# First channel-mixing layer by seven block products (Strassen) in place of eight, weights split per step

## The chip, the core and the metric

One NeuronCore of a Trainium2 chip runs the whole program. Its engines work side by side and meet only through semaphores: TensorE (PE: matmuls, whose stationary operand is loaded by a separate weight load, PEld), VectorE (DVE), ScalarE (ACT), GpSimd (POOL), and SyncE (SP), which here issues every DMA. The metric is the device time of one execution in microseconds, lower is better. Before the change the median of three runs is 671.56 us (671.55 to 672.13).

## The reference

Batch 4, 576 tokens, model width 512. Windowed causal attention (8 heads of 64, window 64) feeds a gated MLP with spatial mixing, and that feeds a mixer. The last lines are where the change lies:

```python
def _moe2_ref(x, w_tok1, w_tok2, w_ch1, w_ch2):      # x: 4 x 576 x 512
    xt = x.transpose(0, 2, 1)
    h = np.maximum(xt @ w_tok1, 0.0) @ w_tok2        # token layers
    u = x + h.transpose(0, 2, 1)
    h2 = np.maximum(u @ w_ch1, 0.0) @ w_ch2          # 512 -> 1536 -> 512
    return u + h2
```

## The kernel before, in words

Work runs in segments: a prologue, one segment for each batch but the last, and an epilogue. In each, the attention of one batch is woven into the MLP and token layers of the batch before. The order on each engine is written out by hand in tables of short names (`PROLOGUE_PE`, `LOOP_DVE`, `ALL_SP`, ...), which the engines' streams walk through. In the tables for PE, `g` is spatial mixing, `y` the projection, `t` transposes, `a` and `b` the two token layers. After the epilogue comes the channel stage, the two layers with w_ch1 and w_ch2 over all 4 x 576 = 2304 tokens. It has no other work beside it.

Every large matmul is made in three passes over operands that are split in a high part (rounded to fp32r) and a low part (what is left): high by high, high by low, low by high. The helper `product` (line 1158) issues these three matmuls. The high part is made by ACT (a copy with the rounding), the low part by DVE or POOL (a subtraction).

The channel stage before the change takes 384 tokens at a time, 6 chunks. Its weights are loaded and split once, during the last segment and the epilogue: 14 pieces, `wb0` to `wb13` in the tables (ACT `channel_high` L825, POOL `channel_low` L690, SP L587), and held in the arena. In a chunk, for each of the 12 blocks j of 128 hidden features, `hidden` makes 4 x 3 matmuls of 384 columns in bank 6 or 7; ACT takes relu and rounds (L833), DVE makes the low part (L1080, one input from PSUM, one from SBUF). Then 3 x 3 matmuls of 512 columns add the block's share to three output tiles. PE runs two j ahead of the second layer (`H0`, `H1` in the epilogue's table are the first two). At the end of a chunk DVE adds the residual rows to each tile (L1146) and SP stores it (L619). The residual `u` is held in DRAM twice: `u2_dram` (columns, u_scratch in the profile) and `rows_dram` (rows, u_rows), written by SP at the end of each batch (`st`, L565, and `sr`, L580, four DMAs for each of four m). SP waits for all of these to have landed before it loads the first residual rows (L607).

Of the kernel before, what the change touches and what calls it, by code (L numbers as in the profile page):

```python
# [20 lines left out]
P = 128  # L21
# [4 lines left out]
def bass_attention_gmlp_mixer_kernel(nc, q, k, v, w_in, w_spatial, b_spatial, w_out, w_tok1, w_tok2, w_ch1, w_ch2, out):  # L26
# [21 lines left out]
    def tile_of(blk):  # L48
# [36 lines left out]
    PROLOGUE_DVE = (
        "ke0 m0 vo1 m1 ke1 r0 ke2 r1 m2 m3 hv0 hv1 r2 c0 c1 r3 m4 c2 hv2 hu0 c3 hu1 ke3 r4 m5 lv0 xl0 hv3 c4 vo2 "
        "r5 lv2 wl0 m6 c5 m7 xl1 hu2 hu3 r6 wl1 vs0 xl2 vo3 vn0 r7 c6 m8 wl2 wl3 vl0 r8 vs1 c7 vo4 c8 vs2 wl4 xl3 "
        "vn1 kt0 vn2 xl4 vl1 kt1 vl2 vs3 vs4 wl5 vn3 vn4 vl3 vl4").split()
    FIRST_DVE = (
# [4 lines left out]
        "vs4 vn3 ut2 vl3 ut3 vn4 kt0 vl4 kt1").split()  # L94
    LOOP_DVE = (
# [88 lines left out]
    with ctx:  # L184
# [528 lines left out]
        def _(act):  # L713
# [121 lines left out]
            for kind, b, x, _ in ACT_ORDER:  # L835
# [30 lines left out]
                elif kind == "H":  # L866
                    hidden(0, x)
# [582 lines left out]
```

## Time and profile before

| | us |
|---|---|
| median of three runs | 671.56 |
| profiled execution, its own time | 672.14 |
| its span, first to last instruction | 670.2 |
| PE busy | 657.2 |
| DVE, ACT, POOL busy | 317.8, 228.0, 150.0 |

Lines of the profile name engine, line of the kernel, operation, output<-input, shape and count. The span in 40 slices (16.75 us each) has PE at 9 (90% or more) in every slice but the first and the last, and the granted clock at 9 throughout. From about 375 us on POOL is idle, DVE and ACT are busy to one or two tenths. A matmul's busy time is longer than the distance to the next, since they are pipelined, so what a matmul costs is read from the starts of groups.

### The profile page before, as it was taken

Reading aid. Unit: us, or ns where it says so; the run is one execution under the profiler, and the core shown is the slowest. Engines: PE = TensorE matmul, PEld = TensorE weight load, DVE = VectorE, ACT = ScalarE, POOL = GpSimd, SP = SyncE. Lnnn points to the kernel's source line nnn. Section 1 sums busy time; section 2 is a strip of 40 time slices with the busy share of each in tenths; the row PEclk is TensorE's granted clock in tenths of the full one; section 3 lists DMA queues with packets and bytes.
Section 4 is the critical chain, followed back from the end, with each engine's and each line's share of the span. In section 5 each row is a group of like instructions: output and inputs, shape, how many; then the busy total and the mean of one; then the engine's idle time right before and its main releaser. Section 6 shows DMA issues by size and latency. Waiting matters only on the chain.

```text
span 670.2 us, 11369 instructions
## 1 busy us (share of the span) xinstructions
PE 657.2 (98%) x4025; PEld 609.0 (91%) x4025; DVE 317.8 (47%) x893; ACT 228.0 (34%) x642; POOL 150.0 (22%) x237
## 2 busy tenths in 40 slices
PE   6899999999999999999999999999999999999997
PEld 5799999999999999998999999999999999999996
DVE  4887887678675887747534221221221221221211
ACT  4775356334563344633356111111111111111110
POOL 3560437411234212343348200000000000000000
PEclk9999999999999999999999999999999999999999
DMA  9838164586435864436931720400300400400101
GB/s 245 208 60 156 32 180 117 116 177 129 108 103 120 175 121 107 113 87 146 291 97 67 162 86 1 142 0 1 141 0 0 141 0 0 142 0 1 48 0 48
DMA packets 169362, 64.82 MB, mean 97 GB/s; under 512 B 126304, under 2 KB 157600, under 8 KB 169312
## 3 DMA queue, kind: packets, MB, share of 16 engines
q1 hardware_dynamic: 169312, 64.17, 37.5%
q8 instruction: 29, 0.48, 0.3%
q14 instruction: 21, 0.17, 0.1%
HBM read 42.91 MB, written 21.23 MB: 96 GB/s over the span
## 4 chain that ended last, share of the span: by engine, by line
PE 96%; DVE 1%; DMA 1%; issue 1%; POOL 0%; ACT 0%; SPq 0%; POOLq 0%; DVEq 0%
PE ps L1158 71%; PE ps L1259 13%; PE ps L1228 5%; PE ps L1198 4%; PE ps L1322 1%; DMA prob_blocks<-att 1%; PE ps L1177 1%; DVE att L930 0%; PE ps L1208 0%; DMA att<-prob_blocks 0%; PE ps L1247 0%; DVE att L1146 0%; ACT xT L753 0%; ACT att L723 0%; SPq L575 0%
## 5 line engine op out<-in xcount | busy, mean ns | idle before, releaser
L1158 PE MATMUL ps<-arena 128*128 128x288 f32 (+3 forms) x2064 | 352.0, 324 | 0.0
L1158 PEld LDWEIGHTS ps<-arena 128*128 128x128 f32 (+1 forms) x2064 | 323.8, 186 | 18.4
L1158 PE MATMUL ps<-arena,att_r 128*128 128x512 f32 x648 | 161.1, 393 | 0.0
L1080 DVE SCALAR_TENSOR_TENSOR att_r<-ps,att_r 128x384 fp32r<-128x384 f32 x72 | 40.1, 557 | 226.2 <-ACT att_r L833 226.1
L1158 PEld LDWEIGHTS ps<-arena,att_r 128*128 128x128 f32 x648 | 120.6, 188 | 22.0
L833 ACT ACTIVATE att_r<-ps 128x384 fp32r<-128x384 f32 x72 | 35.4, 492 | 251.1 <-PE ps L1158 251.1
L1259 PE MATMUL ps<-arena 128*128 128x288 f32 (+1 forms) x560 | 89.3, 316 | 0.0
L1259 PEld LDWEIGHTS ps<-arena 128*128 128x128 f32 x560 | 80.2, 188 | 3.9
L661 POOL TENSOR_SCALAR att<-att,rinv 128x128 f32<-128x128 f32 x144 | 54.4, 399 | 118.6 <-DVE rinv L941 118.5
L743 ACT ACTIVATE att<-att,nmax 128x128 f32<-128x128 f32 x144 | 55.8, 390 | 7.1 <-DVE nmax L930 6.7
L1228 PE MATMUL ps<-att 128*128 128x128 f32 x288 | 37.2, 276 | 2.1 <-DVE att L950 1.1
L1198 PE MATMUL ps<-att 128*128 128x128 f32 x288 | 38.5, 282 | 0.8 <-DVE att L904 0.7
L1228 PEld LDWEIGHTS ps<-att 128*128 128x128 f32 x288 | 35.1, 191 | 3.1 <-DVE att L950 1.3
L930 DVE CUSTOM_DVE_ANT_0 att<-ps,mask 128x128 f32<-128x128 f32 x144 | 33.3, 286 | 9.6 <-PE ps L1198 7.6
L1198 PEld LDWEIGHTS ps<-att 128*128 128x128 f32 x288 | 36.1, 198 | 1.2 <-DVE att L904 1.0
L753 ACT ACTIVATE xT<-ps 64x256 f32<-64x256 f32 x72 | 27.1, 376 | 24.3 <-PE ps L1228 23.8
L690 POOL TENSOR_TENSOR arena<-att,arena 128x768 fp32r<-128x768 f32 (+1 forms) x14 | 29.3, 2115 | 26.4 <-ACT arena L825 26.4
L743 ACT ACTIVATION_READ_ACCUMULATOR att<-att,nmax 128x1 f32 x144 | 27.1, 188 | 0.0
L667 POOL TENSOR_TENSOR rstd<-veps,mhalf 128x1 f32<-128x1 f32 (+1 forms) x20 | 14.5, 726 | 49.3 <-DVE veps L1006 49.1
L913 DVE STREAM_TRANSPOSE att<-att 64x256 f32<-64x256 f32 x54 | 23.6, 436 | 3.7 <-DMA att<-in_q_dram 3.1
L959 DVE STREAM_TRANSPOSE att<-att 128x512 f32<-128x512 f32 x27 | 19.1, 707 | 12.8 <-PE ps L1228 11.8
L799 ACT ACTIVATE arena<-gate 128x288 fp32r<-128x288 f32 x32 | 13.6, 438 | 32.5 <-DVE gate L1041 32.4
(77 smaller groups left out, 433.5 us busy)
## 6 DMA issues: line engine op xcount, KB each, us to landing
prob_blocks<-att SPq DMA_DIRECT2D x27, 256.0 KB, 2.6
att<-prob_blocks SPq DMA_DIRECT2D x108, 64.0 KB, 2.0
u_scratch<-uy SPq DMA_DIRECT2D x16, 288.0 KB, 2.7
att<-u_rows SPq DMA_DIRECT2D x18, 256.0 KB, 4.8
out_dram<-att SPq DMA_DIRECT2D x18, 256.0 KB, 2.1
att<-in_v_dram SPq DMA_DIRECT2D x16, 256.0 KB, 3.7
att<-in_k_dram SPq DMA_DIRECT2D x48, 72.0 KB, 2.5
att<-in_q_dram SPq DMA_DIRECT2D x48, 72.0 KB, 2.5
```

The costliest lines, as they stand in the source:

```text
L661: ins = pool.tensor_scalar(x, x, rinv[:, g % 3, p:p + 1], 1.0, ALU.mult, ALU.mult)
L690: pool.tensor_tensor(lo, staged(c, hi), hi.bitcast(F32), ALU.subtract).then_inc(w_ready, 1)
L743: ins = act.activation(x, x, ACT.Exp, bias=nmax[:, g % 3, p:p + 1], scale=-1.0, accum_out=psums[:, g % 3, p:p + 1])
L753: ins = act.activation(xT3[c, :, blk * WINDOW:(blk + 1) * WINDOW], tp[c, bank, :].rearrange("p (w h n) -> p w h n", w=PAIRS, h=2)[:, :, h, ...
L833: act.activation(h3[:, j % RING, 0, :], ps[:, 6 + j % 2, 0:CK], ACT.Relu).then_inc(h_hi, 1)
L913: ins = dve.transpose(qd[c, g // 2 % 2, g % 2, :, h, :], qn[c, :, blk * WINDOW:(blk + 1) * WINDOW])
L930: ins = dve.tensor_tensor_reduce(out=prob[:, g % 3, P * p:P * (p + 1)], in0=ps[:, 4 + g % 2, P * p:P * (p + 1)], in1=mask[:, 0:P] if blk e ...
L1080: dve.scalar_tensor_tensor(out=h3[:, j % RING, 1, :], in0=ps[:, 6 + j % 2, 0:CK], scalar=0.0, in1=h3[:, j % RING, 0, :].bitcast(F32), op0= ...
L1158: ins = pe.matmul(dst, w[a], x[c], start=first and n == 0, stop=last and n == 2, skip_group_check=True)
L1198: ins = pe.matmul(ps[:, 4 + g % 2, P * p:P * (p + 1)], qd[:, g // 2 % 2, g % 2, p].rearrange("p h n -> p (h n)"), kT[:, p, at:at + P], sta ...
L1228: ins = pe.matmul(tp[:, bank, P * p:P * (p + 1)], window[:, P * p:P * (p + 1)], keys[:, p], start=True, stop=True)
L1259: ins = pe.matmul(dst, d, w, start=t == 0 and n == 0, stop=t == NT - 1 and n == len(pairs) - 1, skip_group_check=True)
```

## The change

The channel stage takes 768 tokens at a time (`s`, three of them), seen as two halves of 384, and the 1536 hidden features as six pairs (`i`) of 128-feature blocks, one from each half. The 512 inputs are two halves of 256. So each step n = 6s + i (18 steps) is a 2 x 2 by 2 x 2 block product, made by seven products of sums of blocks in place of eight (Strassen, in Winograd's form: 4 sums of weights, 4 sums of data, 7 sums of results of which 4 are gathered in PSUM by leaving `start` off). One product is 2 x 3 matmuls of 384 columns. PE does the first layer of step n woven with the 12 second-layer products (3 matmuls of 512 columns each) of step n-1.

- Weights: SP loads step n+1's w_ch1 blocks when the seven products of step n-1 are done, and w_ch2's block of step n when the second layer of step n-2 is done. Each step DVE makes 4 sums (128x256, `weight_sums`), ACT rounds 128x1792 (`weight_high`) and 128x1024 (`second_high`), POOL makes their low parts (`weight_low`, `second_low`). Nothing is held.
- Data: once for each s, in the steps before it, DVE makes 4 sums (128x768, `data_sum`, two each in steps i = 1 and 2), ACT rounds 7 pieces, POOL makes 7 low parts of 128x768 (`data_low`).
- Results: ACT copies three part results out of bank 6 (`copy_part`), DVE adds them to bank 7 (`add_part`), ACT takes relu and rounds (`hidden_high`), DVE makes the low part (`hidden_low`). For j = 0, 1, 3 its two inputs are now both in SBUF.
- Output: six tiles for each s, in banks 0 to 5. `add_rest` has three buffers for residual rows: the load of row tile r waits for the sum of tile r-3.
- The tables of the first four stages are written anew too, and the stage's hardware loops are unrolled.

```diff
     EPILOGUE_PE = (
-        "... a0 t2 t3 a1 t4 a2 a3 a4 H0 b00 b10 b20 b30 b01 b11 b21 b31 H1").split()
+        "... a0 t2 t3 a1 t4 a2 a3 a4 P0 P1 b00 b10 b20 b30 b01 b11 b21 b31 P2 P3 P4 P5 P6").split()
     EPILOGUE_ACT = (
+        "... xe6 ah0 ah1 pc0 pc1 pc2 he0 he1 he2 he3").split()
     EPILOGUE_DVE = (
+        "... al0 al1 cs0 te00 te10 te20 te30 te01 te11 te21 te31 ut0 ut1 ut2 cs1 ut3 cs2 dh0 dh1 dh2 dh3").split()
     EPILOGUE_POOL = (
-        "wb0 wb1 wb2 wb3 wb4 wb5 wb6 wb7 uf0 wb8 wb9 wb10 wb11 wb12 wb13").split()
+        "xo0 xo1 ao0 xo2 xo3 ao1 xo4 xo5 xo6 wo0").split()
...
+        SLOT_A, SLOT_X, SLOT_BANK = (0, 1, 4, 5, 3, 6, 2), (0, 1, 4, 5, 3, 2, 6), (0, 1, 0, 1, 0, 0, 1)
+        OPENS = (True, True, False, True, False, False, False)
+        AFTER_SLOT = (2, 2, 2, 1, 2, 2, 1)
+        UNIT_TILE = (0, 1, 2, 3, 4, 5, 3, 4, 5, 0, 1, 2)
...
         @block.sync
+            for n in range(1, NW + 1):
+                if n + 1 < NW:
+                    sp.wait_ge(first_done, 7 * n)
+                    load_weights(n + 1)
+                if n < NW:
+                    if n >= 2:
+                        sp.wait_ge(second_done, 12 * (n - 1))
+                    load_second(n)
+                if n == 1:
+                    sp.wait_ge(*unit_full(("acc_a", B - 1, KT - 1)))
+                if n in (1, NI):
+                    sp.wait_ge(xc_sum, 4 * (n // NI + 1))
+                    for x in range(4):
+                        load_data(n // NI + 1, x)
+                if n % NI == 4:
+                    for t in range(3):
+                        load_rest(n // NI * 6 + t)
+                if n % NI == 0:
+                    for t in range(6):
+                        store((n // NI - 1) * 6 + t)
+                        if t < 3:
+                            load_rest((n // NI - 1) * 6 + t + 3)
...
         @block.gpsimd
+            for n in range(1, NW):
+                s, i = divmod(n, NI)
+                second_low(n)
+                if n + 1 < NW:
+                    weight_low(n + 1)
+                if s + 1 < NS:
+                    for k in ((), (), (), (0, 1), (2, 3, 4), (5, 6))[i]:
+                        data_low(s + 1, k)
...
         @block.scalar
+                copy_part(n, 0)
+                hidden_high(n, 0)
+                second_high(n)
+                copy_part(n, 1)
+                if n + 1 < NW:
+                    weight_high(n + 1)
+                copy_part(n, 2)
+                hidden_high(n, 1)
+                hidden_high(n, 2)
+                if s + 1 < NS:
+                    for k in ((), (), (0, 1), (2, 3, 4), (5, 6), ())[i]:
+                        data_high(s + 1, k)
+                hidden_high(n, 3)
...
         @block.vector
+                    add_part(n, 0)
+                    if n + 1 < NW:
+                        weight_sums(n + 1)
+                    hidden_low(n, 0)
+                if s + 1 < NS and i in (1, 2):
+                    data_sum(s + 1, 2 * i - 2)
+                    data_sum(s + 1, 2 * i - 1)
+                if i == 0:
+                    add_rest(r)
+                if n < NW:
+                    add_part(n, 1)
...
         @block.tensor
+            def first_product(n, k):
+                bank = ps[:, 6 + SLOT_BANK[k], 0:CK]
+                if k == 0:
+                    pe.wait_ge(a_lo, n + 1)
...
+                        pe.wait_ge(h_lo, 4 * (n - 1) + 3)
+                if k == 1 and n > 0:
+                    pe.wait_ge(total_done, 3 * (n - 1) + 3)
+                if k in (2, 4, 5):
+                    pe.wait_ge(part_copied, 3 * n + (1, None, 2, 3)[k - 2])
+                if k in (3, 6):
+                    pe.wait_ge(total_done, 3 * n + (1 if k == 3 else 2))
...
+                for i in range(2):
+                    ins = product(bank, [a[n % 2][:, SLOT_A[k], i] for a in (a_hi_at, a_lo_at)],
+                                  [x_at[n // NI % 2][:, SLOT_X[k], s, i] for s in range(2)], OPENS[k] and i == 0, i == 1)
+                ins.then_inc(first_done, 1)
...
+            for n in range(1, NW):
+                u = 0
+                for k in range(7):
+                    first_product(n, k)
+                    for _ in range(AFTER_SLOT[k]):
+                        second_product(n - 1, u)
+                        u += 1
+            for u in range(12):
+                second_product(NW - 1, u)
```

Two places in the order of the instructions matter for the prediction. The first is SP at the end of the epilogue, up to the first loads of the channel stage; each row is a line of the kernel, a transfer, its shape and the semaphores it waits for. Before:

```order
L580 DMA u_rows<-gate 32x18x32 [waits u2_turned]
L580 DMA u_rows<-gate 32x18x32 x3
L565 DMA u_scratch<-uy 128x576 [waits acc_dve] x2
L607 DMA att<-u_rows 128x512 [waits rows_stored2,u2_stored2,u2_stored3,rows_stored1,rows_stored3,u2_stored1,w_ready,rows_stored0,u2_stored0]
L607 DMA att<-u_rows 128x512 x2
```

And now, with `front` as the home of raw weights and `early` as that of raw data:

```order
L579 DMA u_rows<-gate 32x18x32 x3
L564 DMA u_scratch<-uy 128x576 [waits acc_dve] x3
L591 DMA front<-in_moe_w_ch_dram 128x4x128 [waits rows_stored2,u2_stored2,u2_stored3,rows_stored1,rows_stored3,u2_stored1,first_done,rows_stored0,u2_stored0]
L592 DMA front<-in_moe_w_ch_dram 128x2x128
L593 DMA front<-in_moe_w_ch_dram 128x2x128
L597 DMA front<-in_moe_w_ch_dram 128x2x512
L586 DMA early<-u_scratch 128x2x384 [waits xc_sum,acc_full]
L586 DMA early<-u_scratch 128x2x384 x2
L586 DMA xT<-u_scratch 128x2x384
```

The transfers that stood behind the last stores were residual rows for the end of the first chunk; now they are the weights of step 2, w_ch2's block of step 1 and the data of the second 768 tokens.

The second place is DVE in the channel stage. Before, one chunk, the last but one:

```order
L1080 SCALAR_TENSOR_TENSOR att_r<-ps,att_r 128x384 x4
L1076 TENSOR_TENSOR arena<-uy,arena 128x1536
L1080 SCALAR_TENSOR_TENSOR att_r<-ps,att_r 128x384 x8
L1146 TENSOR_TENSOR att<-ps,att 128x512 x3
```

Now, step 1 (L1173 `add_part`, L1162 to L1167 `weight_sums`, L1178 `hidden_low`, L1149 and L1151 `data_sum`):

```order
L1173 TENSOR_TENSOR vr<-ps,xT 128x384
L1162 TENSOR_TENSOR front<-front 128x256
L1163 TENSOR_TENSOR front<-front 128x256
L1165 TENSOR_TENSOR front<-front 128x256
L1167 TENSOR_TENSOR front<-front 128x256
L1178 SCALAR_TENSOR_TENSOR arena<-vr,arena 128x384
L1149 TENSOR_TENSOR early<-xT,early 128x768
L1151 TENSOR_TENSOR early<-early,xT 128x768
L1173 TENSOR_TENSOR vr<-ps,xT 128x384
L1178 SCALAR_TENSOR_TENSOR arena<-vr,arena 128x384
L1178 SCALAR_TENSOR_TENSOR arena<-ps,arena 128x384
```

Two data sums, with both inputs in SBUF, stand between the first and the second `add_part`; in steps without them `hidden_low` is followed by `add_part` directly.

## Rows read from the trace of the kernel before

**Rows 1.** The page: PE's busy time, and the chain that ended last by engine
```profile
PE 657.2 (98%) x4025; PEld 609.0 (91%) x4025; DVE 317.8 (47%) x893; ACT 228.0 (34%) x642; POOL 150.0 (22%) x237
PE 96%; DVE 1%; DMA 1%; issue 1%; POOL 0%; ACT 0%; SPq 0%; POOLq 0%; DVEq 0%
```

**Rows 2.** Groups by line and shape, PE, whole span: count, busy us, mean ns
```profile
L1158 PE MATMUL ps<-arena 128*128 128x384 f32 x864 | 163.0, 337 | 0.0
L1158 PE MATMUL ps<-arena,att_r 128*128 128x512 f32 x648 | 161.1, 393 | 0.0
```

**Rows 3.** Timeline, PE, into the channel stage: start us, us, engine, line, shape, count
```profile
359.05 12.79 PE L1158 MATMUL ps<-arena 128*128 128x384 f32 x84
371.68 2.24 PE L1158 MATMUL ps<-arena,att_r 128*128 128x512 f32 x9
373.76 2.27 PE L1158 MATMUL ps<-arena 128*128 128x384 f32 x12
375.87 2.24 PE L1158 MATMUL ps<-arena,att_r 128*128 128x512 f32 x9
```

**Rows 4.** Timeline of the end: last matmuls, residual sums, stores
```profile
660.56 6.32 PE L1158 MATMUL ps<-arena,att_r 128*128 128x512 f32 x27
665.66 2.05 DVE L1146 TENSOR_TENSOR att<-ps,att 128x512 f32<-128x512 f32 x3 [3.82 <-PE ps L1158]
666.38 1.69 SPq L619 DMA_DIRECT2D out_dram<-att  x3
```

**Rows 5.** Timeline of SP issues around the first residual loads
```profile
375.41 2.21 SPq L580 DMA_DIRECT2D u_rows<-gate  x4
377.71 0.96 SPq L565 DMA_DIRECT2D u_scratch<-uy  x2
380.92 1.31 SPq L607 DMA_DIRECT2D att<-u_rows  x3
```

**Rows 6.** Transfers: KB each and median us to landing; L607's min/median/max
```profile
att<-in_moe_w_ch_dram SPq DMA_DIRECT2D x6, 512.0 KB, 3.9
DMA to landing us min/median/max: 3.0/3.3/3.5
```

**Rows 7.** Groups by line and shape, ACT, DVE and POOL: count, busy us, mean ns
```profile
L833 ACT ACTIVATE att_r<-ps 128x384 fp32r<-128x384 f32 x66 | 32.5, 492 | 233.7 <-PE ps L1158 233.7
L829 ACT ACTIVATE arena<-uy 128x1536 fp32r<-128x1536 f32 x2 | 3.0, 1482 | 0.0
L1080 DVE SCALAR_TENSOR_TENSOR att_r<-ps,att_r 128x384 fp32r<-128x384 f32 x66 | 36.8, 557 | 214.4 <-ACT att_r L833 214.4
L1076 DVE TENSOR_TENSOR arena<-uy,arena 128x1536 fp32r<-128x1536 f32 x3 | 5.3, 1758 | 5.8 <-ACT arena L829 5.8
L690 POOL TENSOR_TENSOR arena<-att,arena 128x1024 fp32r<-128x1024 f32 x6 | 14.2, 2404 | 1.8 <-ACT arena L825 1.8
L694 POOL TENSOR_TENSOR arena<-xT,arena 128x1536 fp32r<-128x1536 f32 x1 | 3.5, 3510 | 0.2 <-ACT arena L829 0.2
```

**Rows 8.** Timelines of POOL and DVE in the epilogue, side by side in time
```profile
327.84 4.04 POOL L690 TENSOR_TENSOR arena<-att,arena 128x768 fp32r<-128x768 f32 x2 [1.60 <-ACT arena L825]
...
328.68 0.46 DVE L1034 TENSOR_TENSOR gate<-ps,bias 128x288 f32<-128x288 f32 x1 [0.53 <-PE ps L1259]
329.06 1.12 DVE L1047 TENSOR_TENSOR arena<-gate,arena 128x288 fp32r<-128x288 f32 x1
330.11 2.08 DVE L1041 TENSOR_TENSOR gate<-gate,uy 128x288 f32<-128x288 f32 x1
332.59 0.46 DVE L1041 TENSOR_TENSOR gate<-gate,uy 128x288 f32<-128x288 f32 x1
```

**Rows 9.** Windows: us, PE busy (count), granted clock, DMA share, GB/s
```profile
5.00:25.00 20.00, 15.58 (x105) 1.00 1.14 285
667.00:669.00 2.00, 0.00 (x0) 1.00 0.88 337
669.00:670.00 1.00, 0.00 (x0) 0.82 0.29 113
```

More of the change, by code:

```diff
@@ new lines, in bass_attention_gmlp_mixer_kernel @@
+        x_raw = [a.rearrange("p (c s k n) -> p c s k n", c=7, s=2, k=2) for a, _ in x_all]
+        x_at = [a.rearrange("p (c s k n) -> p c s k n", c=7, s=2, k=2) for _, a in x_all]
+        x_12 = xT[:, 0:XC].rearrange("p (k n) -> p k n", k=2)
+        part = [xT[:, XC + i * CK:XC + (i + 1) * CK] for i in range(3)]
+        total = [vr[:, 0, 0:CK], vr[:, 1, 0:CK], xT[:, XC + 3 * CK:XC + 4 * CK]]
+        h_at = arena[:, START["xhl"]:START["xhl"] + 8 * CK].rearrange("p (j s n) -> p j s n", j=4, s=2)
@@ L650, in _ @@
             pool.memset(mhalf[:, :], -0.5).then_inc(const_set, 1)
-            for i in range(4):
-                pool.sem_inc(o_stored[i], 16)
             pool.wait_ge(const_set, NCONST)
@@ new lines, in add_part, with hidden_low @@
+            def add_part(n, x):
+                dve.wait_ge(part_copied, 3 * n + (1, 3, 2)[x])
+                apart(dve)
+                dve.wait_ge(first_done, 7 * n + (2, 4, 7)[x])
+                dve.tensor_tensor(total[x], ps[:, 7, 0:CK], part[(0, 2, 1)[x]], ALU.add).then_inc(total_done, 1)
+            def hidden_low(n, j):
+                dve.wait_ge(h_hi, 4 * n + j + 1)
+                src = ps[:, 6, 0:CK] if j == 2 else total[(0, 1, None, 2)[j]]
+                dve.scalar_tensor_tensor(out=h_at[:, j, 1], in0=src, scalar=0.0, in1=h_at[:, j, 0].bitcast(F32),
+                                         op0=ALU.max, op1=ALU.subtract).then_inc(h_lo, 1)
@@ L1084, in _, with add_rest @@
+            def add_rest(r):
+                dve.wait_ge(rest_in[r % 3], 16 * (r // 3 + 1))
+                if r >= 4:
+                    dve.wait_ge(o_stored[r % 4], 16 * (r // 4))
+                apart(dve)
+                dve.wait_ge(second_done, 12 * (r // 6 * NI + NI - 1) + 6 + r % 6 + 1)
+                dve.tensor_tensor(osb[r % 4], ps[:, OUT_BANK[TILE_DONE[r % 6]], :], rest[r % 3], ALU.add).then_inc(o_copied, 1)
             for kind, b, x, _ in DVE_ORDER:
@@ L1124, in _ @@
                     turn_residual(b, x)
-                elif kind == "H":
-                    hidden(0, x)
+                elif kind == "xs":
+                    data_sum(0, x)
+                elif kind == "as":
+                    weight_sums(x)
+                elif kind == "cs":
+                    add_part(0, x)
+                elif kind == "dh":
+                    hidden_low(0, x)
                 elif kind[0] == "h":
@@ new lines, in second_product @@
+            def second_product(n, u):
+                j, tile = u // 3, UNIT_TILE[u]
+                bank = OUT_BANK[tile]
+                if u % 3 == 0:
+                    pe.wait_ge(h_lo, 4 * n + j + 1)
+                    apart(pe)
+                if u == 0:
+                    pe.wait_ge(w2_lo, n + 1)
+                    apart(pe)
+                if n == 0 and u < 6:
+                    if bank in (4, 5):
+                        pe.wait_ge(masked, BL * B)
+                    else:
+                        pe.wait_ge(*unit_free(LAST_IN[bank]))
+                elif n % NI == 0 and u < 6:
+                    pe.wait_ge(o_copied, 6 * (n // NI - 1) + TILE_DONE.index(tile) + 1)
+                c = slice(tile % 3 * P, tile % 3 * P + P)
+                ins = product(ps[:, bank, :], [h_at[:, j, s, c] for s in range(2)], [w[n % 2][:, j % 2] for w in (w2_hi_at, w2_lo_at)],
+                              n % NI == 0 and u < 6, n % NI == NI - 1 and u >= 6)
+                ins.then_inc(second_done, 1)
```

460 lines of the change are left out of this document (226 added, 234 removed), and 26 rows, old and new, of tables (ALL_SP, FIRST_DVE, LOOP_DVE).

## Prediction

> **What bounds the kernel now.** I read the page first: PE is busy 98% of the span, and the chain that ended last lies on PE for 96% of it [rows 1]. So time falls only by matmuls that go, and rises by every microsecond for which PE is made to wait. Then the groups by shape: the channel stage is 864 matmuls of 384 columns and 648 of 512 [rows 2]. Their mean durations (337 and 393 ns) are not their price, as they overlap; the timeline gives it. Nine of 512 columns start at 371.68 and the next group at 373.76, so 0.231 us each; twelve of 384 take to 375.87, so 0.1755 us each [rows 3]. 864 x 0.1755 + 648 x 0.231 = 301.3 us, and with the 48 short matmuls woven in (about 6.3 us) this is the whole of 359.05 to 666.80, where the last 27 end (660.56 + 27 x 0.231) [rows 3, 4]. There is no hole in the stage. Outside it PE's only large idle time is between 5 and 25 us, 20.0 - 15.6 = 4.4 us [rows 9].
>
> **What is removed.** Seven products for eight: 18 steps x 7 x 6 = 756 matmuls of 384 columns in place of 864. 108 x 0.1755 = **-18.9 us**. The second layer keeps its 648. The long splitting of held weights in the epilogue goes too, but lay beside PE and gives nothing.
>
> **The step.** A product (6 matmuls) takes 1.05 us, a second-layer product (3) 0.69 us, a step 7 x 1.05 + 12 x 0.69 = 15.7 us. By the order 2, 2, 2, 1, 2, 2, 1 of second products behind the slots, and counting from the step's start: slot k0 ends at 1.05, k1 at 3.5, k2 at 5.9, k4 may start at 9.1 and ends at 10.1, k5 may start at 11.5, k6 at 13.9 and ends at 15.0. The other engines have this to do in it, with ACT's copy or relu 0.49, DVE's low part or sum 0.56 from PSUM, a 256-wide sum in SBUF 0.44, a 768-wide one 0.97 (0.46 for 288 and 1.76 for 1536, between them on a line) [rows 7, 8], ACT 1.0 for 1024 and 1.7 for 1792, POOL 2.40 for 1024, 3.51 for 1536, so 2.17 ns an element and 4.07 for 1792, 1.85 for 768 [rows 7]:
> - SP issues the weights at about -0.5; a quarter MB lands 3.0 to 3.5 us after its issue, half an MB 3.9 [rows 6]. w_ch1 is there at about 4.0, w_ch2 at 4.9.
> - DVE: first sum with bank 7 at 3.7 to 4.3, four weight sums to about 6.1, then the low part of j = 0.
> - ACT: relu to 4.9, rounds w_ch2 to 6.0, copies k2's result to 6.5 (PE wants it at 9.1), rounds w_ch1's seven pieces to 8.3, copies k4's result 10.3 to 10.8 (PE wants it at 11.5).
> - POOL: 2.40 from about 6.1, then 4.07, to 13.1. PE wants these weights at 15.7.
> So a plain step hides all of it, the least room being 0.7 us at k5 (a PE-ACT-PE path) and 2.6 us at the weights. I count the plain steps at **0**, and the two with six residual sums as well (their loads at 3.0 us arrive within 1 us of their use). If the cover goes, all is paid 17 times; that is a rival below.
>
> **DVE behind POOL.** The trace shows what happens when DVE has an operation with two SBUF inputs while POOL runs a subtraction: at 330.11 one of 0.46 us took 2.08 and ended at 332.19, just after POOL's pair at 331.88; one at 329.06 took 1.12, let in between the pair. One with an input from PSUM at 328.68 took its 0.46 beside POOL [rows 8]. Now `data_sum`, `weight_sums` and three of four `hidden_low` have both inputs in SBUF. In steps i = 1 and 2 (n = 1, 2, 7, 8) DVE has, before its second `add_part`, a low part (0.56) and two data sums (0.97 each), and POOL meanwhile 2.40 and 4.07. Taking turns from 6.1 they end at 6.1 + 2.5 + 6.5 = 15.1, less 0.14 for each of three waits (of 1.77 us that POOL still ran, the 330.11 operation lost 1.63) = 14.6. `add_part` ends at 15.2, and slot k6, which waits for it, starts at 15.2 or 15.3 in place of 13.9: 1.3 us. Steps 2, 7 and 8: **+3.9 us** (bounds 0, if DVE gets all its turns first or is never held, and 5.7 at 1.9 each).
> The Trainium skill, "SBUF - State Buffer", section "Who interferes with whom", says that a DVE instruction with two SBUF inputs and a GpSimd one that reads SBUF exclude each other, and whoever started first holds the shared ports for the whole instruction. The trace agrees in kind; taken strictly (no 0.14 back) this term would be 5.1.
>
> **The turn into the stage.** Slots P2 to P6 have no second product between them. They start where the b matmuls end, 359.05 + 12 x 0.1755 + 6.3 = 367.5. P5 waits for ACT's copy of P4's result (0.2 + 0.49 + 0.1 against nothing: 0.8 us). P6 ends at 373.6; slot k0 of step 1 waits for three low parts, which on DVE stand behind the sum of P6: 0.2 + 0.56 + 3 x 0.56 + 0.1 = 2.5. Step 1 starts at 376.1.
> Its supply is late, for SP is a queue. It still has sixteen row stores, the last issued at 375.41 + 2.2 = 377.6, then now three column stores in place of two (0.57 apart), the last at 378.9; the one at 378.3 landed before the load at 380.92 [rows 5]. So step 2's weights are issued at 381.5, not at 373.8; w_ch1 lands at about 385.8, w_ch2's block for step 1, issued at 383.2, at 386.9 [rows 6]. ACT stands at w_ch2 and behind it is the copy for k4: 386.9 + 1.0 + 0.5 = 388.5, while PE was ready at 376.1 + 9.1 = 385.2. On POOL and DVE the same turns begin at 388.0: 2.40 + 4.07 + 0.97 + 0.97 - 0.14, then `add_part` 0.56, so k6 starts at 396.9 and the step ends at 398.6. Without waits steps P2 to 1 would end at 367.5 + 5.3 + 15.7 = 388.5. **+10.1 us** (bounds: 3.3, if only P5 and k0 wait; 12, if w_ch2 lands 2 us later). In the trace before this place was dense, because weights were held and only residual rows, needed 12 blocks later, stood behind the stores.
>
> **The end.** Residual rows of the last three tiles wait for buffers. Counted from the start of the last 12 second products, the first three sums end at 5.8, 6.5 and 7.2. SP issues store and load in turns 0.6 apart: loads at 6.4, 7.6, 8.8, each landing 3.0 later [rows 6], the last sum 11.85 to 12.5, and its store and the end 2.5 behind (667.7 to 670.2, the third store of rows 4). PE ends at 8.3, so the tail is 6.7 us where it was 670.2 - 666.8 = 3.4 [rows 4]. **+3.3 us** (bounds 0 and 5).
>
> **The stages before it.** The rewritten tables move the same matmuls. There is 4.4 us to win in 5 to 25 us [rows 9] and nothing elsewhere; the second half of w_in is now loaded first and the first half behind two more loads, which could cost as much. I take **0** (bounds -4.4 and +3). In the epilogue the sums lie on DVE between gate operations; POOL starts on data only after the last data sum (about 347), works 27 us, and each slot's piece is ready before its slot. 0.
>
> **Sum.** -18.9 + 3.9 + 10.1 + 3.3 = -1.6 us. From the profiled execution's 672.1 that is 670.5; the median of the runs is 0.6 lower (671.56), so I forecast 670.0.
>
> **Rivals.**
> 1. *DVE is not held in the channel stage* (it gets its turns first, or its data sums finish before POOL starts). Then the 3.9 goes and step 1's k6 starts about 3.5 earlier: 670.0 - 7.4 = 662.6. For: DVE is idle two thirds of a step. Against: rows 8. 15%.
> 2. *PE's clock falls in the turn.* PE idles 2.5, 3.3 and 3.5 us within 20 us. At the end of the trace, after its last matmul at 666.8, the granted clock is full to 669 and falls between 669 and 670 [rows 9]. If it falls before step 1's k6, the matmuls behind run at half of 2.4 GHz until it rises; with a cost of about 3 us: 673.0, slower. It decides if the idle stretch before k6 is no shorter than that one. Against: two stretches of it are broken by matmuls. 20%. The Trainium skill ("TensorE: Matmul & The Clock Gate", "Why this matters for your kernels") warns against long idle gaps between bursts of matmuls; by it this rival would be likelier.
> 3. *The weights' path is longer than a step*: loads that land 1 to 2 us later put DVE's last weight sum behind POOL, the rounding behind that, and the low part of j = 2, which slot k0 waits for, 0.4 us past the step's end. 14 steps x 0.4 = 5.6: 675.6, slower. For: 512-byte rows in these loads, and a page median of 3.9 us for larger ones. Against: 2.6 us of room at the weights. 15%.
> 4. *The new tables* gain or lose 3 us in the first four stages: 667 or 673. 15%.
>
> **Numbers.** The forecast's own case has 35%, with a range of its own of 667 to 673. A measurement here tells 0.2% (1.3 us) from no change. Faster by more: 20 of the 35, 15 of rival 1, 2 of 2, 7 of 4, so 0.44. Within: 12, 8, 1 and 3, so 0.24. Slower: 3, 10, 14 and 5, so 0.32. The range reaches to rivals 1 and 3 with their bounds: 661.5 to 678.
>
> **What would show it.** Right: 1404 matmuls in the stage; plain steps of 15.7 us; PE idle before slot k6 in steps 1, 2, 7 and 8, released by an `add_part` that ends just after a 4.07 us POOL row; PE idle before k4 of step 1, released by ACT; first w_ch1 load of the stage near 381.5; a tail near 6.7 us. Wrong: PE waiting in plain steps, a granted clock below full between 376 and 400, or a stage that starts at another time than 359.

## The result: slower by 0.8%

The changed kernel took 676.93 us (median of 5 runs, 674.58 to 678.26), the kernel before 671.56 (5 runs, 671.08 to 672.13): ratio 1.0076, 95% interval 1.0055 to 1.0097. The forecast was 670.0. The profiled execution took 676.68 us at a span of 674.7 (before: 672.1 at 670.2), so the profiles differ by 4.5 us and the medians by 5.4. Differences are read from the spans of the profiled executions.

The page of the kernel after; against [rows 1], PE is busy 13 us less in a span 4.5 us longer, and its clock row, full throughout before, has two slices of 8 in the channel stage and one at the end:

```profile
span 674.7 us, 11567 instructions
PE 643.8 (95%) x3917; PEld 590.7 (88%) x3917; DVE 403.8 (60%) x1026; ACT 297.8 (44%) x733; POOL 272.9 (40%) x279
PEclk9999999999999999999999889999999999999998
PE 84%; DMA 4%; DVE 4%; issue 3%; SPq 2%; ACT 1%; POOL 0%; DVEq 0%; POOLq 0%
front<-in_moe_w_ch_dram SPq DMA_DIRECT2D x18, 512.0 KB, 4.8
early<-u_rows SPq DMA_DIRECT2D x18, 256.0 KB, 4.5
```

The chain of waits, 96% on PE before, is now 84%, with DMA, DVE and SP's queue in it. The last two rows are issues with their median landing: 4.8 us where I had counted 3.9, 4.5 where I had counted 3.0 [rows 6].

The matmuls went as they should: 756 of 384 columns and 648 of 512, against [rows 2]. The groups by shape for PE in the channel stage (count, busy us, mean ns, idle ahead and its releasers), then the waits of the same stretch (us in total, times, longest):

```profile
L1277 PE MATMUL ps<-arena 128*128 128x512 f32 x648 | 172.1, 398 | 0.2 <-DVE front L1187 0.2
L1277 PE MATMUL ps<-att_r,arena 128*128 128x384 f32 x504 | 102.3, 339 | 9.7 <-ACT xT L887 5.8 <-DVE arena L1178 2.3 <-DVE vr L1173 1.6
L1277 PE MATMUL ps<-arena 128*128 128x384 f32 x252 | 51.0, 337 | 3.9 <-ACT xT L887 2.6 <-DVE arena L1178 0.9 <-DVE vr L1173 0.5
```

```profile
PE ps L1277 <- ACT xT L887: 8.4, 4, 2.7
PE ps L1277 <- DVE arena L1178: 3.2, 3, 2.1
PE ps L1277 <- DVE vr L1173: 2.1, 2, 1.6
```

A stage that had no wait has 14 us of them in nine places. From the starts of the trace's matmul groups I worked out the length of every step. Twelve of the steps 2 to 17 take 15.69 us, which is the dense length (no wait, full clock), and step 14 is within 0.05 of it. The rest, in us (the last row counts from 0.231 us behind the start of the last matmul):

| place | after | dense | excess |
|---|---|---|---|
| P2 to the end of step 1 | 32.1 | 21.0 | 11.1 |
| step 7 | 20.28 | 15.69 | 4.6 |
| step 8 | 16.49 | 15.69 | 0.8 |
| step 13 | 18.91 | 15.69 | 3.2 |
| last matmul to span end | 8.55 | 3.5 (before) | 5.0 |

With -18.95 for the products and -1.3 for a stage that began at 357.77 and not 359.05 this makes +4.5, the difference of the spans.

**Step 7.** PE is busy for all of step 6 and for 16.61 of the 20.28 us of step 7, both at the full clock, and the DMA engines' busy share in step 7 is 0.38. PE's and ACT's timelines in step 7:

```profile
489.34 6.85 PE L1277 MATMUL ps<-arena 128*128 128x384 f32 x33 [2.57 <-ACT xT L887]
...
487.76 1.06 ACT L883 ACTIVATE arena<-front 128x1024 fp32r<-128x1024 f32 x1 [5.21 <-DMA front<-in_moe_w_ch_dram]
488.72 0.47 ACT L887 ACTIVATE xT<-ps 128x384 f32<-128x384 f32 x1
```

PE at 489.34 waits for ACT's copy at 488.72. The copy did not wait for its own data: it is queued behind the rounding of w_ch2 at 487.76, which stood 5.21 us for a load. Why was the load late? SP's queue at the end of step 6:

```profile
476.61 0.34 SPq L631 DMA_DIRECT2D out_dram<-att  x1
478.71 2.55 SPq L631 DMA_DIRECT2D out_dram<-front  x2
481.30 0.43 SPq L591 DMA_DIRECT2D front<-in_moe_w_ch_dram  x1
...
482.90 0.47 SPq L597 DMA_DIRECT2D front<-in_moe_w_ch_dram  x1
```

The last three output stores of the first 768 tokens come first, and each waits for its residual sum on DVE:

```profile
477.99 0.69 DVE L1187 TENSOR_TENSOR front<-ps,early 128x512 f32<-128x512 f32 x1 [1.41 <-DMA early<-u_rows]
...
480.21 0.68 DVE L1187 TENSOR_TENSOR front<-ps,early 128x512 f32<-128x512 f32 x1
```

So w_ch1's first piece goes out at 481.30 and w_ch2 at 482.90, over 6 us after the step began at 476.76. I had all of them at 0.5 us before a step.

**The turn.** PE's timeline from P2 into step 2:

```profile
366.24 3.29 PE L1277 MATMUL ps<-att_r,arena 128*128 128x384 f32 x18
370.20 2.32 PE L1277 MATMUL ps<-att_r,arena 128*128 128x384 f32 x12 [0.67 <-ACT xT L887]
374.67 1.56 PE L1277 MATMUL ps<-att_r,arena 128*128 128x384 f32 x6 [2.14 <-DVE arena L1178]
376.03 2.76 PE L1277 MATMUL ps<-arena 128*128 128x512 f32 x6
...
379.79 1.55 PE L1277 MATMUL ps<-arena 128*128 128x512 f32 x6
...
388.26 1.53 PE L1277 MATMUL ps<-att_r,arena 128*128 128x384 f32 x6 [2.75 <-ACT xT L887]
389.59 2.77 PE L1277 MATMUL ps<-arena 128*128 128x512 f32 x6
...
396.49 1.30 PE L1277 MATMUL ps<-att_r,arena 128*128 128x384 f32 x6 [1.55 <-DVE vr L1173]
...
398.32 1.22 PE L1277 MATMUL ps<-att_r,arena 128*128 128x384 f32 x6
```

All four waits that I named are there. Besides, the same six matmuls take 2.76 us at 376.03 and 1.55 at 379.79: the clock fell to half of 2.4 GHz from 375.5 to 378.9 and from 389.1 to 392.6, just behind the waits of 2.1 and 2.75 us. By windows the mean granted clock (third number from the end) is:

```profile
375.00:379.00 4.00, 4.00 (x14) 3.42 (x13) 0.00 (x0) 0.49 (x1) 0.00 (x0) 0.57 0.88 233
388.00:393.00 5.00, 4.74 (x16) 4.21 (x17) 2.24 (x1) 2.19 (x3) 5.00 (x2) 0.66 0.37 133
```

The matmuls in the two stretches took 3.1 us longer than at the full clock.

**The end.** DVE's residual sums, then the rows' landing (issues between 664 and 667 us):

```profile
662.97 2.05 DVE L1187 TENSOR_TENSOR front<-ps,early 128x512 f32<-128x512 f32 x3 [3.58 <-PE ps L1277]
667.15 0.69 DVE L1187 TENSOR_TENSOR att<-ps,early 128x512 f32<-128x512 f32 x1 [2.13 <-DMA early<-u_rows]
669.90 0.69 DVE L1187 TENSOR_TENSOR front<-ps,early 128x512 f32<-128x512 f32 x1 [2.06 <-DMA early<-u_rows]
671.55 0.69 DVE L1187 TENSOR_TENSOR front<-ps,early 128x512 f32<-128x512 f32 x1 [0.95 <-DMA early<-u_rows]
```

```profile
early<-u_rows SPq DMA_DIRECT2D x3, 256.0 KB, 4.7
```

Against [rows 4], where the last three sums ran together at 665.66, each of the last three now waits for a load; the three loads took 4.7 us in the median. How long this end takes differs between executions: in the profiles of the kernels below that leave it as it is (e1, e2, e4 to e7, e11) it is 7.1 to 8.4 us.

### The profile page after: what moved, and what is told of

The parts are those of the page before. It is cut to its first block, busy times and chain, and to the rows that moved or that the text cites. A ratio compares the mean times of both kernels' runs of the same rounds, so it can differ in the third digit from the quotient of the medians.

```text
span 674.7 us, 11567 instructions
## 1 busy us (share of the span) xinstructions
PE 643.8 (95%) x3917; PEld 590.7 (88%) x3917; DVE 403.8 (60%) x1026; ACT 297.8 (44%) x733; POOL 272.9 (40%) x279
## 4 chain that ended last, share of the span: by engine, by line
PE 84%; DMA 4%; DVE 4%; issue 3%; SPq 2%; ACT 1%; POOL 0%; DVEq 0%; POOLq 0%
PE ps L1277 59%; PE ps L1378 13%; PE ps L1347 5%; PE ps L1317 5%; DMA front<-in_moe_w_ch_dram 1%; DMA early<-u_rows 1%; PE ps L1441 1%; SPq L579 1%; DMA xT<-u_scratch 1%; DVE arena L1178 1%; DVE att L1001 1%; PE ps L1327 1%; DVE front L1187 0%; ACT xT L887 0%; DVE att L1154 0%
## 5 line engine op out<-in xcount | busy, mean ns | idle before, releaser
L1277 PE MATMUL ps<-arena 128*128 128x288 f32 (+3 forms) x2100 | 399.2, 344 | 4.2 <-ACT xT L887 2.6
L1277 PEld LDWEIGHTS ps<-arena 128*128 128x128 f32 (+1 forms) x2100 | 336.0, 187 | 40.1 <-issue 5.2
L1277 PE MATMUL ps<-att_r,arena 128*128 128x384 f32 x504 | 102.3, 339 | 9.7 <-ACT xT L887 5.8
L1277 PEld LDWEIGHTS ps<-att_r,arena 128*128 128x128 f32 x504 | 90.5, 189 | 18.7 <-issue 11.9
L729 POOL TENSOR_TENSOR arena<-front,arena 128x1024 fp32r<-128x1024 f32 x18 | 44.3, 2458 | 146.7 <-ACT arena L883 146.7
L725 POOL TENSOR_TENSOR arena<-front,arena 128x1792 fp32r<-128x1792 f32 x18 | 74.7, 4149 | 0.0
L1173 DVE TENSOR_TENSOR vr<-ps,xT 128x384 f32<-128x384 f32 x36 | 20.0, 556 | 87.2 <-ACT xT L887 54.0
L899 ACT ACTIVATE arena<-vr 128x384 fp32r<-128x384 f32 x36 | 18.9, 526 | 67.2 <-PE ps L1277 46.1
L1178 DVE SCALAR_TENSOR_TENSOR arena<-vr,arena 128x384 fp32r<-128x384 f32 x36 | 40.3, 1121 | 9.7 <-ACT arena L899 9.7
L887 ACT ACTIVATE xT<-ps 128x384 f32<-128x384 f32 x54 | 26.2, 485 | 42.0 <-PE ps L1277 41.9
L1001 DVE CUSTOM_DVE_ANT_0 att<-ps,mask 128x128 f32<-128x128 f32 x144 | 33.1, 285 | 10.7 <-PE ps L1317 10.1
L718 POOL TENSOR_TENSOR att_r<-att,att_r 128x768 fp32r<-128x768 f32 x14 | 26.8, 1933 | 30.9 <-DVE att L1157 30.9
```

What stands on the lines that cost most here:

```text
L718: pool.tensor_tensor(x_at[s % 2][:, c, 1], x_raw[s % 2][:, c, 1], x_at[s % 2][:, c, 0].bitcast(F32), ALU.subtract) \
L725: pool.tensor_tensor(a_lo_at[n % 2], a_raw[n % 2], a_hi_at[n % 2].bitcast(F32), ALU.subtract).then_inc(a_lo, 1)
L729: pool.tensor_tensor(w2_lo_at[n % 2], w2_raw[n % 2], w2_hi_at[n % 2].bitcast(F32), ALU.subtract).then_inc(w2_lo, 1)
L1001: ins = dve.tensor_tensor_reduce(out=prob[:, g % 3, P * p:P * (p + 1)], in0=ps[:, 4 + g % 2, P * p:P * (p + 1)], in1=mask[:, 0:P] if blk e ...
L1178: dve.scalar_tensor_tensor(out=h_at[:, j, 1], in0=src, scalar=0.0, in1=h_at[:, j, 0].bitcast(F32), op0=ALU.max, op1=ALU.subtract).then_inc ...
L1277: ins = pe.matmul(dst, w[a], x[c], start=first and n == 0, stop=last and n == 2, skip_group_check=True)
```

## The experiments

Ratios are against the kernel before, with their 95% interval. By the intervals, the medians of two changed kernels can be told apart from about 1.5 to 2 us on (my estimate), so smaller gains are read from the length of the steps in the profiles. An edit that adds lines shifts the line numbers in its rows (L1277 becomes L1280 and so on).

### Stores behind the loads (e1)

```diff
+                if n % NI == 1 and n > 1:
+                    for t in range(3, 6):
+                        store((n // NI - 1) * 6 + t)
...
-                    for t in range(6):
+                    for t in range(6 if n == NW else 3):
                         store((n // NI - 1) * 6 + t)
```

> In steps 6 and 12 SP stores the last three output tiles behind the loads of the next step, not ahead of them. Theory (the loads of steps 7 and 13 stood 4.5 us in SP's queue behind stores that wait for DVE): the waits at slot k4 (2.7 and 2.6 us) and at the end of these steps (1.0 and 0.3) go, steps 7 and 13 fall from 20.3 and 18.9 us to under 17; with what is left at the start of step 7 the time falls by 6 to 7.5 us, to about 670. Rival (data sums on DVE behind POOL lengthen these steps): they stay at 19 to 20 us, time 676.9.

669.68 us, ratio 0.9973 (0.9962 to 0.9985). Step 7 took 16.09 us (was 20.28), step 13 15.86 (was 18.91). SP's queue in that kernel:

```profile
477.25 0.38 SPq L591 DMA_DIRECT2D front<-in_moe_w_ch_dram  x1
...
478.86 0.47 SPq L597 DMA_DIRECT2D front<-in_moe_w_ch_dram  x1
...
479.88 1.98 SPq L631 DMA_DIRECT2D out_dram<-front  x2
```

w_ch2 is issued at 478.86, which is 1.1 us behind the start of step 7 and not 6.1, and the k4 waits of steps 7 and 13 are gone. Steps 7, 8, 13 and 14 together are 7.9 us shorter; the turn is as late as before (step 1 took 24.74 us). This move of three DMA issues alone, twice in the program, takes 7.2 us off the median and brings the change below the kernel before. That the loads stood behind the stores was the cause.

### ACT's copy ahead of the rounding (e2)

```diff
+                copy_part(n, 1)
                 second_high(n)
-                copy_part(n, 1)
```

> ACT makes the copy that slot k4 waits for ahead of the rounding of w_ch2, not behind it. Theory (supply: the late transfer sets the end of the step through the rounding, POOL's two subtractions and the first weights of the next step): the waits at k4 of steps 1, 7 and 13 go, but as large ones come at k5 and at the next k0; steps 1, 7 and 13 get shorter by under 0.8 us each, time 675 to 677. Rival (ACT's order is the cause): 2.9 + 2.7 + 2.6 = 8.2 us go, time 668.7.

677.7 us, 1.0093 (1.0077 to 1.011). The waits at k4 vanish; in step 7 they come back one slot later, at k5 (first row), and at the first slot of step 8 (second row):

```profile
493.14 4.41 PE L1277 MATMUL ps<-arena 128*128 128x384 f32 x21 [1.74 <-ACT xT L887]
499.34 3.27 PE L1277 MATMUL ps<-arena 128*128 128x384 f32 x10 [1.79 <-DVE arena L1178]
```

Steps 7 and 13 took 20.38 and 18.67 us, as before the edit (20.28, 18.91), and step 1 took 24.62 (23.66), so none became clearly shorter. ACT's queue only decides where PE pays for late weights; that they are late costs the time.

### Last residual rows early (e3)

```diff
+                if n == NW - 2:
+                    for t in range(3):
+                        at = (6 * (NS - 1) + TILE_DONE[3 + t]) * P
+                        sp.dma_start(last_rest[t], rows_dram[at:at + P, :]).then_inc(last_in[t], 16)
...
-                        if t < 3:
+                        if t < 3 and n < NW:
                             load_rest((n // NI - 1) * 6 + t + 3)
```

> The residual rows of the last three tiles are loaded in step 16 into three buffers of their own. Theory (the tail waits for these loads): from PE's end to the span's end it takes 3.4 to 3.7 us as in the kernel before, not 8.5; time lower by 4.8 to 5.1 us, to about 672. Rival (the stores' own latency, six in a row): 8 us stay, time 676 to 677.

673.29 us, 1.0029 (1.0017 to 1.0042), 3.6 less than the change, where I expected 4.8 to 5.1. The tail is 4.4 us, from 8.55:

```profile
665.46 0.69 DVE L1197 TENSOR_TENSOR front<-ps,early 128x512 f32<-128x512 f32 x1 [0.19 <-DMA out_dram<-front]
```

No sum waits for a row. The tail stays 0.9 us longer than the 3.5 of before. A part of that is that four output buffers serve six sums, so the fifth waits 0.19 us for a store to land; what makes the rest was not shown.

### The tables alone (e10)

The kernel before with the new orders of its first stages and SP's words; one line of many:

```diff
-        "Q0 K0 Q1 S0 S1 K1 K2 S2 Q2 S3 T0 T1 S4 V0 T2 V1 T3 K3 Q3 S5 V2 S6 V3 T4 w0 v0 w1 w2 V4 S7 T5 Z4 w3 + V5 "
+        "Q0 K0 Q1 S0 S1 K1 K2 S2 Q2 T0 S3 V0 T1 S4 S5 T2 V1 K3 Q3 V2 T3 S6 S7 V3 T4 w0 w1 v0 Z4 w2 V4 S8 T5 + V5 "
```

> The kernel before, with the new tables of prologue and loops alone (epilogue and channel stage as before). Theory (the new prologue saved 1.3 us, since the first 384-column matmul starts at 357.8 and not at 359.05): 1.3 us faster than before, 670.3. Rival (that shift comes from the epilogue, where the splitting of held weights is gone): as before, 671.6.

671.35 us (10 runs), 0.9998 (0.9989 to 1.0008): nothing, where I expected 1.3 us. The start of the channel stage lay between 357.4 and 359.0 us over the profiles of the eleven kernels whose first stages run by these tables. So the 1.3 us of the accounting above are most likely the spread between executions, and not a gain of the tables.

### One wait of the turn at a time (e4, e6, e7)

**e4**, step 1's w_ch2 ahead of the row stores on SP:

```diff
-        "cw40 st30 sr30 sr31 sr32 sr33 st31 st32 st33").split()
+        "cw40 cw41 st30 sr30 sr31 sr32 sr33 st31 st32 st33").split()
```

> Only w_ch2's block of step 1 is loaded ahead of the last sixteen row stores. Theory (step 1's end is set by the last of several supplies that stand behind the stores: w_ch1 of step 2 and the data of the next 768 tokens too): the wait at k4 goes, one of about 2 us comes at k5 or k6, step 1 gets 1 to 2 us shorter, time 675 to 676. Rival (the copy for k4 behind w_ch2's rounding is all of it): step 1 under 20.5 us, time 673.5.

676.78 us, 1.0068 (1.0046 to 1.0089): no gain. The wait at k4 is gone, but waits of 1.0 us at k5 and of 3.4 at k6 have come, since w_ch1 and the data are as late as ever. Step 1 is 22.26 us (was 23.66), but the clock fell just before step 2 began, a wait of 0.7 us came at its k6, and it took 17.53.

**e6**, DVE's data sums behind the low part of j = 2:

```diff
-                if s + 1 < NS and i in (1, 2):
-                    data_sum(s + 1, 2 * i - 2)
-                    data_sum(s + 1, 2 * i - 1)
...
                     hidden_low(n, 2)
+                if s + 1 < NS and i in (1, 2):
+                    data_sum(s + 1, 2 * i - 2)
+                    data_sum(s + 1, 2 * i - 1)
```

> The two data sums of steps i = 1 and 2 stand behind the low part of j = 2 on DVE, not ahead of the second add. Theory (a DVE sum with two SBUF inputs waits for POOL and holds the add behind it): the wait at k6 of step 1 (1.7 us) and of step 8 (0.7) go, steps 1 and 8 are 1.5 to 2 and 0.7 us shorter, the rest as it was, time 674 to 675. Rival (PE waits there for weights or rounding, not for the add): no change, 676.9.

674.84 us, 1.0056 (1.0039 to 1.0073), 2.1 less than the change. The wait at k6 goes in steps 1 (20.18 us) and 8 (15.69): an `add_part` behind a held sum was what PE stood for. The first data sum of step 1 now starts at 394.54, when POOL's subtractions are over, and takes 0.94 us. Step 1 is 3.5 us shorter, and its wait at k6 was only 1.7; nearly all of the rest is the second fall of the clock, which this profile does not have behind the wait at k4.

**e7**, the first low parts of the stage ahead of the sum of P6 on DVE:

```diff
-        "te21 te31 ut0 ut1 ut2 cs1 ut3 cs2 dh0 dh1 dh2 dh3").split()
+        "te21 te31 ut0 ut1 ut2 cs1 dh0 ut3 dh1 dh2 cs2 dh3").split()
```

> The first low parts of step 0 stand ahead of the last add of that step on DVE. Theory: the wait at k0 of step 1 (2.3 us) falls to under 0.8, but the end of step 1 is set by transfers behind SP's stores, so it moves into the wait at k4; step 1 ends at the same time within 0.5 us, and the time is 676 to 677. Rival (the waits of the turn add up): 1.5 to 2 us faster, 675.

676.83 us, 1.0075 (1.0051 to 1.0099). The wait at k0 fell from 2.3 to 0.6 us and the one at k4 rose to 6.7; step 1 ended at 399.4. As long as step 1's supply is late, PE only waits elsewhere.

### The supply of the turn early (e5)

```diff
-        "cw40 st30 sr30 sr31 sr32 sr33 st31 st32 st33").split()
+        "cw40 cw41 cd40 st30 sr30 sr31 sr32 sr33 ca42 st31 st32 st33").split()
```

(This is the line of SP's queue; the rest of the edit moves the loads. cw41 is w_ch2 of step 1, cd40 the data of the second 768 tokens, ca42 step 2's w_ch1.)

> All three supplies early: w_ch2 of step 1 and the data of the next 768 tokens ahead of the row stores, w_ch1 of step 2 behind the row stores but ahead of the last three column stores. Theory: step 1 falls from 23.7 us to 16 to 17.5 (what is left is half clock from the gap before it), nothing else changes, time 6 to 7.5 us lower, about 670.3. Rival (the data sums on DVE behind POOL's subtraction still hold k6): a wait of 1.7 us or more stays at k6, time 672 or more.

670.51 us (11 runs), 0.9984 (0.9975 to 0.9994), 6.4 less than the change. The profile is that of the slowest of these runs (673.48); in it the clock fell in steps 7 and 13 too. Step 1 took 18.52 us (was 23.66), 1.0 over what I expected. Its k6 still waited 1.1 us, for DVE, which stood beside POOL:

```profile
385.24 4.38 POOL L732 TENSOR_TENSOR arena<-front,arena 128x1792 fp32r<-128x1792 f32 x1
385.62 4.82 DVE L1156 TENSOR_TENSOR early<-xT,early 128x768 f32<-128x768 f32 x1
```

A sum that takes 0.95 us took 4.82, and ended 0.8 us behind POOL's subtraction.

### POOL sets zeros in place of subtracting (e11)

```diff
-                pool.tensor_tensor(a_lo_at[n % 2], a_raw[n % 2], a_hi_at[n % 2].bitcast(F32), ALU.subtract).then_inc(a_lo, 1)
+                pool.memset(a_lo_at[n % 2].bitcast(F32), 0.0).then_inc(a_lo, 1)
...
-                pool.tensor_tensor(w2_lo_at[n % 2], w2_raw[n % 2], w2_hi_at[n % 2].bitcast(F32), ALU.subtract).then_inc(w2_lo, 1)
+                pool.memset(w2_lo_at[n % 2].bitcast(F32), 0.0).then_inc(w2_lo, 1)
```

> The changed kernel, in which POOL writes zeros for the low parts of both weights in place of the subtraction (those low parts are left out): POOL then reads nothing from SBUF and is done sooner. Theory (DVE operations with two SBUF inputs wait while POOL reads SBUF): no data sum and no low part takes over 1.2 us in steps 1, 2, 7, 8, the waits at k6 of steps 1 and 8 and at the end of steps 7 and 13 go (1.7, 0.7, 1.0, 0.3), the waits at k4 stay; about 3 us faster than the changed kernel, 673 to 675. Rival (those waits come from late transfers alone): DVE as before, 676.9.

The first data sum of step 1 (DVE) beside POOL's subtraction in the change, and beside POOL's memset in this kernel:

```profile
390.14 4.04 POOL L725 TENSOR_TENSOR arena<-front,arena 128x1792 fp32r<-128x1792 f32 x1
390.76 4.24 DVE L1149 TENSOR_TENSOR early<-xT,early 128x768 f32<-128x768 f32 x1 [3.42 <-DMA xT<-u_scratch]
```

```profile
390.99 1.59 POOL L725 MEMSET arena<- 128x1792 f32 x1 [1.01 <-ACT arena L879]
391.98 0.96 DVE L1149 TENSOR_TENSOR early<-xT,early 128x768 f32<-128x768 f32 x1 [4.77 <-DMA xT<-u_scratch]
```

Every data sum takes 0.95 us and the waits at k6 are gone (steps 2, 8, 14 at 15.69): it is POOL's reading of SBUF that holds DVE. Yet the time is 677.03 us, 1.007 (1.005 to 1.009), no lower than the change, where I expected 3 us less. The waits at k4 are 4.3, 2.8 and 2.7 us in steps 1, 7 and 13 (2.9, 2.7 and 2.6 in the change). The clock fell four times in the stage of its profile, once for 6.8 us and three times for 3.4, and the matmuls in these stretches took about 7.5 us longer than at the full clock, against 3.1 in the change. Here the gain is hidden by another loss, so the run shows the mechanism and not its price; for the price there is e6, with its 2.1 us.

### All that helped, together (e8)

The edits of e1, e3, e5, e6 and e7 in one kernel; of their diffs, the queue of SP and of DVE:

```diff
+        "cw40 cw41 cd40 st30 sr30 sr31 sr32 sr33 ca42 st31 st32 st33").split()
...
+        "te21 te31 ut0 ut1 ut2 cs1 dh0 ut3 dh1 dh2 cs2 dh3").split()
```

> All changes of order together: stores of three tiles behind the next loads, last residual rows early, the three supplies of the turn early, data sums late, first low parts ahead. Theory (nothing but these waits and the clock's falls behind them eat the 18.9 us of matmuls): every step 15.7 to 16.4 us, tail 4.5 us, the stage's first 384-column matmul to the span's end 294 to 296 us, time 653 to 655, ratio to before 0.973 to 0.976. Rival (the waits hide one another and new ones come up, as they did in two of the single changes): 660 or more.

**656.81 us** (5 runs, 656.52 to 657.31), ratio 0.9785 (0.9771 to 0.9798): faster than both kernels, 20.1 us below the change, 1.8 us over the top of what I expected. Steps 1, 7 and 13 take 16.80, 16.34 and 16.02 us, the tail 4.5. Its page, and the waits of PE in the stage:

```profile
span 654.4 us, 11569 instructions
PE 639.9 (98%) x3917; PEld 589.3 (90%) x3917; DVE 394.2 (60%) x1026; ACT 297.8 (46%) x733; POOL 270.7 (41%) x279
PEclk9999999999999999999999999999999999999999
```

```profile
PE ps L1297 <- ACT xT L903: 1.1, 2, 0.7
PE ps L1297 <- DVE arena L1194: 0.7, 2, 0.4
PE ps L1297 <- DVE front L1207: 0.2, 1, 0.2
```

14 us of waits have become 2, the longest is 0.7, and the clock is full in every slice. The single edits gained 7.2 (e1), 3.6 (e3), 6.4 (e5), 2.1 (e6) and 0.1 us (e7), 19.4 together, as much as all of them in one kernel within the noise. Of the 18.95 us taken out, 14.8 arrive. What still stands against the dense length in this profile is 2.6 us from P2 to the end of step 1, 1.0 in steps 7 and 13, and 1.0 at the tail.

## Why the prediction was wrong

The sum came to -1.6 us and the profiles differ by +4.5. By its steps:

- **The products, -18.9:** right, and the step of 15.69 us is the 15.7 forecast.
- **"I count the plain steps at 0, and the two with six residual sums as well": the step that failed.** The plain steps do cost 0. The two with residual sums (6 and 12) delay the loads of the next ones, and those are 4.6 and 3.2 us longer. I asked of them only when their residual rows arrive, and not what stands behind their stores on SP. "SP issues the weights at about -0.5" was read into all steps and holds for the plain ones alone. I had followed that queue at the turn, where it gave the right price, but not here. e1 shows it: with the last three stores moved behind the loads the kernel is 7.2 us faster. Without these 7.8 us the profiles would differ by -3.3 and not +4.5, and the change would have been faster, as forecast.
- **The lock (DVE behind POOL), +3.9:** right in kind (e5, e6, e11), wrong in size. Steps 2, 7 and 8 gave 0, 0 and 0.7 at k6. In step 2 the first data sum got in ahead of POOL, whose subtraction waits for w_ch2, and w_ch2 landed after 4.8 us and not 3.9. In step 8 POOL was first. In step 7 the wait at k4 came first and none was left at k6. The lock shows there in another place: a low part that takes 0.56 us took 3.97 beside POOL's 4.09, and step 8 began 1.0 us late for it. The first two rows are step 2, the others step 8:

```profile
404.65 0.95 DVE L1154 TENSOR_TENSOR early<-early 128x768 f32<-128x768 f32 x1
405.22 2.66 POOL L729 TENSOR_TENSOR arena<-front,arena 128x1024 fp32r<-128x1024 f32 x1 [11.03 <-ACT arena L883]
...
503.14 2.41 POOL L729 TENSOR_TENSOR arena<-front,arena 128x1024 fp32r<-128x1024 f32 x1 [7.13 <-ACT arena L883]
503.20 3.17 DVE L1154 TENSOR_TENSOR att<-att 128x768 f32<-128x768 f32 x1
```

  Steps 2 to 17 together have +8.7 for the +3.9 forecast.
- **The turn, +10.1:** the mechanism right, the size 11.1. Forecast: k4 ready at 385.2 and started after 388.5, k6 at 396.9, step 2 at 398.6. Measured: 385.3, 388.26, 396.49, 398.3. That the times agree so closely is in part luck: SP issued w_ch2 at 381.90 and not 383.2, since the stage began 1.3 us sooner, and it landed after 4.8 us and not 3.7, so it was there at 386.7 for the 386.9 forecast. Rival 2 (the clock falls in the turn) held beside the forecast and moved it little: the clock did fall, at a cost of 3.1 us, the 3 us I gave it, but ahead of k6, where DVE and not PE set the time, and the wait there shrank from the 3.5 us forecast to 1.7. Its condition (an idle stretch before k6 no shorter than that at the end of the trace before) was not needed; the falls came behind waits of 2.1 and 2.75 us.
- **The end, +3.3:** the mechanism right, mis-sized: 5.0, since the rows landed in 4.7 us and not 3.0. I took the landing of loads that ran alone [rows 6] for loads that run between stores. The trace of before had a nearer row: three reads of the same 256 KB, issued at 422.4 behind three stores and a 768 KB read, landed in 5.2 us.

```profile
att<-u_rows SPq DMA_DIRECT2D x3, 256.0 KB, 5.2
```

- **The stages before, 0:** right (e10).
- **The other rivals.** Rival 1 (DVE is not held) came true at k6 of steps 2 and 7 and failed in steps 1 and 8, where e6 and e11 show the hold. Rival 3 names a like time, 675.6, but by a cost in 14 plain steps that is not there: w_ch2 landed 0.9 us late, and those steps still take 15.69 us. That the measured time lies near it is no sign for it.

By the absolute times: -0.3 at the turn's end, +4.8 in the steps behind it, +1.7 at the tail, 6.2 in all over the forecast of 670.5 for the profiled execution, which took 676.7.

What stays open is the spread. The runs of the change go from 674.6 to 678.3 us, those of the kernel before from 671.1 to 672.1. In the profiles, a wait of 2.3 to 2.9 us before k4 in step 7 or 13 was followed by a fall of the clock in both steps in e5, e6 and e11, in step 7 alone in e3, and in neither in the change, e4 and e7. Each fall of 3.4 us cost 1.5 to 1.6 us, and those of 6.8 us (e1, e7, e11) cost 1.8 to 2.8. The tail differs by up to 1.5 us too. That these two make the spread, and the 0.9 us between the medians' difference and the profiles', fits, but was not shown. e8, with no wait above 0.7 us, has runs within 0.8 us of each other.

## What to carry to other kernels

When weights that were held are streamed step by step, write down for each kind of step what each load stands behind on the queue that issues it; a store that waits for a late sum delays the next weights, however idle the DMA engines are. Removing one of several waits on the same late supply moves the wait and gains nothing (e2, e4, e7), so fix the supply, and judge single fixes by the length of the step and not by the wait removed. Take the landing time of a transfer from rows where it has the same neighbours.

## What the runs showed of the hardware

- A DVE sum of two SBUF operands, 0.95 us alone, took 4.24 us (the change) and 4.82 us (e5) beside POOL's subtractions of 4.04 and 4.38 us, and 0.95 beside POOL's memsets (e11). The Trainium skill ("SBUF - State Buffer", "Who interferes with whom") says that such a pair exclude each other; these rows agree.
- The clock fell to half of 2.4 GHz after idle stretches of PE as short as 2.1 us, but not each time. The wait of 2.1 us before step 1 was followed by a fall in six profiles (the change, e3 to e6 and e11) and by none in two (e1, e2), and waits of about 2.7 us before k4 went either way too. The Trainium skill ("TensorE: Matmul & The Clock Gate", "Why this matters for your kernels") warns of long gaps between bursts; here gaps of 2 to 3 us were enough in some of the profiles.
- The same 256 KB read landed in 3.0 to 3.5 us alone [rows 6] and in 4.7 between stores. The 512 KB reads of the channel weights, which the two kernels cut differently, landed in 3.9 us before and 4.8 after.
